# VectorE writes the attention's high part of x from the output bank, and the head's side work is spread over its steps

## The reference

```python
scores = scale * np.matmul(q, k.transpose(0, 1, 3, 2))       # 2 batches, 8 heads, 768 tokens, head size 64
keep = is_sink | in_window                                   # 4 sink tokens, window of 128
scores = np.where(keep, scores, -1000000000.0)
a = np.exp(scores - np.max(scores, axis=-1, keepdims=True))
a = a / (np.sum(a, axis=-1, keepdims=True) + 1e-09)
x = matmul(a, v), reshaped to 1536 tokens x 512
h = x @ w_in;  x = np.maximum(0.01 * h, h) @ w_out           # 512 -> 2048 -> 512
h = x @ w_in2; y = (h * (1.0 / (1.0 + np.exp(-h)))) @ w_out2
```

## Time and profile before

| what | before |
|---|---|
| median of three runs | 673.38 us (671.8 to 674.53) |
| the profiled execution's own time | 672.19 us |
| its span in the trace | 669.8 us |
| TensorE busy | 642.4 us, 96% |
| VectorE busy | 278.2 us, 42% |
| ScalarE busy | 299.9 us, 45% |
| GpSimd busy | 119.1 us, 18% |
| head, to the first hidden tile | 68.67 us |

### The profile page before, as it was taken

The page is one execution under the profiler, slowest core; times in us unless marked ns, Lnnn a source line. Parts: engine busy times, 40 slices in busy tenths (PEclk is TensorE's granted clock), DMA queues, the critical chain, the costliest instruction groups (busy, mean ns, idle before and its releaser), DMA issues.

```text
span 669.8 us, 9081 instructions
## 1 busy us (share of the span) xinstructions
PE 642.4 (96%) x3113; PEld 528.3 (79%) x3113; DVE 278.2 (42%) x646; ACT 299.9 (45%) x676; POOL 119.1 (18%) x165
## 2 busy tenths in 40 slices
PE   5989899989989999999999999999999999999997
PEld 3667688877768888887888888888888888888886
DVE  3669555555535555552222225333322222212222
ACT  3778556565536556642333335333322333223332
POOL 4767333242314233310000000000000000000000
PEclk8899999999989999999999999999999999999999
DMA  4664234334331223111011122233211111201101
GB/s 114 174 191 118 81 114 119 111 96 126 97 94 33 79 65 112 32 60 35 1 63 64 64 63 95 94 98 103 103 75 31 64 63 64 95 0 64 64 0 63
DMA packets 16940, 53.27 MB, mean 80 GB/s; under 512 B 2560, under 2 KB 2560, under 8 KB 16896
## 3 DMA queue, kind: packets, MB, share of 16 engines
q1 hardware_dynamic: 16512, 52.63, 25.9%
q10 hardware_dynamic: 384, 0.07, 0.1%
HBM read 49.55 MB, written 3.15 MB: 79 GB/s over the span
## 4 chain that ended last, share of the span: by engine, by line
PE 78%; issue 7%; DVE 5%; ACT 3%; POOL 2%; DMA 2%; POOLq 0%; SPq 0%; ACTq 0%; DVEq 0%
PE h_ps L797 36%; PE y_ps L823 33%; PE o_ps L763 3%; DMA qk_raw<-qk 2%; PE t_ps L731 2%; PE s_ps L718 1%; DVE wout L600 1%; DVE win L594 1%; ACT wout L456 1%; PE y_ps L707 1%; ACT prob L413 1%; DVE g L605 1%; DVE pT L551 1%; POOL k_hl L333 1%; PE t_ps L741 1%
## 5 line engine op out<-in xcount | busy, mean ns | idle before, releaser
L797 PE MATMUL h_ps<-x,win 128*128 128x512 f32 x1152 | 284.6, 394 | 9.1 <-DVE win L594 5.3
L797 PEld LDWEIGHTS h_ps<-x,win 128*128 128x128 f32 x1152 | 214.0, 189 | 54.2 <-DVE win L594 6.9
L463 ACT ACTIVATE g_f<-h_ps 128x512 f32<-128x512 f32 x96 | 57.4, 598 | 268.9 <-PE h_ps L797 268.7
L823 PE MATMUL y_ps<-g,wout 128*128 128x512 f32 x576 | 146.5, 395 | 1.2 <-PE o_ps L763 1.2
L823 PE MATMUL y_ps<-wout,g 128*128 128x512 f32 x576 | 138.2, 389 | 0.0
L600 DVE TENSOR_TENSOR wout<-w_raw,wout 128x512 fp32r<-128x512 f32 x64 | 47.2, 737 | 192.9 <-ACT wout L456 192.9
L823 PEld LDWEIGHTS y_ps<-wout,g 128*128 128x128 f32 x576 | 108.1, 188 | 22.4
L823 PEld LDWEIGHTS y_ps<-g,wout 128*128 128x128 f32 x576 | 103.9, 188 | 20.7 <-issue 1.9
L605 DVE TENSOR_TENSOR g<-g_f,g 128x512 fp32r<-128x512 f32 x96 | 66.0, 687 | 99.9 <-ACT g L465 99.9
L413 ACT ACTIVATE prob<-sm,neg_max 128x260 f32<-128x260 f32 (+1 forms) x96 | 47.0, 490 | 56.5 <-DVE neg_max L543 56.4
L465 ACT ACTIVATE g<-h_ps 128x512 fp32r<-128x512 f32 x96 | 56.9, 593 | 0.0
(11 more groups left out here) (76 smaller groups left out, 415.4 us busy)
## 6 DMA issues: line engine op xcount, KB each, us to landing
w_raw<-w SPq DMA_DIRECT2D x64, 512.0 KB, 3.3
qk_raw<-qk SPq DMA_DIRECT2D x48, 260.0 KB, 4.5
v_raw<-vt SPq DMA_DIRECT2D x12, 256.0 KB, 4.4
y<-qk_raw SPq DMA_DIRECT2D x12, 256.0 KB, 2.3
vs_raw<-vsink ACTq DMA_DIRECT2D x8, 8.0 KB, 4.5
```

Of the source, the lines that this page charges most:

```text
L463: nc.scalar.activation(g_f32[:, F % 2, :], h_ps[:, :], func, alpha=slope)
L797: ins = mm(h_ps[:, :], win[:, split_slot[split_of[F]], wp, c * P:(c + 1) * P], x[:, xp, c, tokens(F)], start=(c == 0 and wp == HI and xp = ...
L823: ins = mm(y_ps[d][:, :], a[:, d * P:(d + 1) * P], r, start=(first and wp == HI and gp == HI), stop=(last and wp == LO))
```

## The change

The high part of x is no longer copied from `att` by ScalarE. VectorE multiplies the output bank by `scale` twice, once into the high part of `x` (two instructions of 64 partitions that write fp32r) and once into `att`; GpSimd waits for both. In the same change:

- the four first weight loads are issued in steps 9, 11, 13 and 15 in place of 4 to 7;
- slice 0 is split in ticks -5 (win) and -3 (wout), and slice 1's win in tick -2, in place of -2, -1 and -1;
- the seven instruction groups on the sink values are set one by one into steps 3 to 9;
- filler is one matmul per step from step 8 on;
- the first half of tile 5's q and k is split in step 19 in place of 18, on ScalarE between the exponential and the first hidden tile's function.

```diff
+    first_loads = (9, 11, 13, 15)
...
-        if s < FT:
+        if s < 2:
+            at, at_out = 3 * s - 5, 3 * s - 3
+        elif s < FT:
             at, at_out = s - 2, s - 1
...
-            return 1 if T < TB else 2
+            return 1 if T < TB else 3 if T == TB else 2
...
-                if PAIRS <= a < 2 * PAIRS:
-                    load_w(a - PAIRS)
+                if a in first_loads:
+                    load_w(first_loads.index(a))
...
-                pool.wait_ge(x_high, e + 1)
+                pool.wait_ge(x_high, 2 * e + 2)
+                pool.wait_ge(att_ready, e + 1)
...
-            def high_x(e):
-                T, half = divmod(e, 2)
-                act.wait_ge(att_ready, e + 1)
-                nc.scalar.activation(x[:, 0, 2 * half:2 * half + 2, T * P:(T + 1) * P], att[:, :, :],
-                                     ACT.Copy).then_inc(x_high, 1)
...
-                if a in scaled_in:
-                    high_x(scaled_in[a])
...
                 if a == FS:
+                    high_qk(T + 1, 0)
                     take_hidden(0)
...
                 wait(dve, x_ready, e)
+                for lo in (0, D):
+                    src = o_bank(e)[lo:lo + D, :].rearrange("p (c n) -> p c n", c=2)[:, :, 2 * lo:2 * lo + P]
+                    nc.vector.tensor_tensor(x[lo:lo + D, 0, 2 * half:2 * half + 2, T * P:(T + 1) * P], src,
+                                            scale[lo:lo + D, :, :], ALU.mult).then_inc(x_high, 1)
...
-            stack_sink_values()
...
+                if 3 <= a < 3 + 5 + B:
+                    stack_sink_values(a - 3)
...
-                    fill(3)
+                    fill(3 if a < 2 * PAIRS else 1)
```

More of the change, by code:

```diff
@@ L503, in _ @@
                 if a == FS:
+                    high_qk(T + 1, 0)
                     take_hidden(0)
-                if a == FS:
                     exp(2 * a + 1)
@@ L518, in _ @@
                     evacuate(F, 0)
-                    if j == j_split(T) and T + 1 < TILES:
-                        high_qk(T + 1, 0)
+                if a > FS and j == j_split(T) and T + 1 < TILES:
+                    high_qk(T + 1, 0)
             for F in range(LAST - FS, NSTEP):
@@ L582, in scale_half @@
             def scale_half(e):
+                T, half = divmod(e, 2)
                 dve.wait_ge(o_done, e + 1)
@@ L621, in evacuate, with stack_sink_values @@
                         nc.vector.tensor_copy(out_sb[:, d, :], y_ps[d][:, :]).then_inc(out_dve, 1)
[L623 to L632, removed]
-                n = H * NS
[L634 to L637, removed]
+            def stack_sink_values(piece):
+                n = H * NS
+                if piece == 0:
+                    dve.wait_ge(vs_loaded, 16 * B * REP)
+                    nc.vector.tensor_copy(vs_hi[:, :, :], vs_raw[:, :, :]).then_inc(vs_step, 1)
+                elif piece == 1:
+                    dve.wait_ge(const_step, CONSTS)
+                    nc.vector.tensor_reduce(block_of[:, :],
+                                            ident[:, :].rearrange("p (r h s) -> p h r s", r=REP, h=H),
+                                            mybir.AxisListType.XY, ALU.add).then_inc(vs_step, 1)
+                elif piece == 2:
+                    dve.wait_ge(vs_step, 1)
+                    nc.vector.tensor_copy(vs_part[:, :, :], vs_hi[:, :, :].bitcast(F32)).then_inc(vs_step, 1)
+                elif piece < 5:
+                    dve.wait_ge(vs_step, 3)
+                    rows = slice((2 * piece - 5) * n, (2 * piece - 4) * n)
                     nc.vector.tensor_tensor(vs_part[rows, :, :], vs_raw[rows, :, :],
                                             vs_hi[rows, :, :].bitcast(F32), ALU.subtract).then_inc(vs_step, 1)
-                dve.wait_ge(vs_step, 5)
-                for b in range(B):
+                else:
+                    b = piece - 5
+                    dve.wait_ge(vs_step, 5)
                     nc.vector.tensor_tensor(vs_st[:, b, :, :],
```

## The result

The changed kernel takes 674.24 us (median of 20 runs, 671.92 to 675.87), the kernel before 672.22 us in as many runs. The ratio is 1.0025, interval 1.0015 to 1.0036: a small loss, 1.7 us by the ratio, clear of no change. The time lies inside the range of the forecast (673.0 us), but on the other side of no change: the forecast stood against 673.38 us as a slight gain. The profiled execution has a span of 672.4 us against 669.8.

What follows compares the result with a forecast made beforehand. TensorE's head was full partly by filler, the others close behind; VectorE would become the bound. Terms -0.1 (head), +0.7 (borders), +0.3 (splitting steps) made +0.9 us on 672.19: 673.1, written 673.0, range 667.5 to 678.5.

Steps and rivals of the forecast that it cites:

- VectorE becomes the bound of the head: Head, steps 9 to 18: VectorE needs about 5.9 us per two steps against 5.30 before, first hidden tile near 70.0.
- blocking: Head: eight VectorE instructions on SBUF wait for GpSimd, 0.35 each in steps 4 to 8, 0.4 after; 3.0 us in all.
- The 48 instructions on x at 0.42 us: VectorE's new instructions for the high part of x read PSUM and scale, so no blocking is added: 0.42 us each.
- The filler buys nothing: Head: with VectorE as bound, the 0.44 us of filler taken from each of eleven steps gains no time.
- The DMA stall goes, since the first weight load is issued four steps later: Head, steps 4 to 8: VectorE's 3.25 us idle piece for the late qk load disappears as loads come one by one.
- In the three steps where q and k are split on the same tick ... taken at +0.1 each: Behind the head: ScalarE up to 0.5 us earlier, GpSimd's x 0.37 later; +0.1 us each, bounds -0.5 and +0.4.
- Block borders: Two borders behind the head where TensorE waits for x: two more instructions, +0.4 us each, 0.7 together.
- I write 673.0: Whole kernel: +0.9 us on the profiled execution's 672.19 gives 673.1, written as 673.0; three runs had a median of 673.38.
- B: Faster rival: VectorE's added work goes into gaps more than allowed, without blocking; about 668 us, chance 0.25.
- C: Slower rival: eight VectorE instructions meet GpSimd's q and k often and wait the full 1.1 us; 679 us, chance 0.12.
- D: Clock rival: with less filler the granted clock falls to 1.2 GHz in the head; +14, 687 us, chance 0.03.
- E: Slower rival: behind the head 0.86 us per half delays masks and g, 16 ticks at 0.3; 678 us, chance 0.10.

Runs made afterwards that it cites:

- the third experiment: Changed kernel with ScalarE's copy of att into x for the eight halves of the head, VectorE's two instructions behind it: 670.93 us, ratio 0.9990 to the kernel before.
- that of the first: Changed kernel with ScalarE's copy of att into x again, all else of the change kept: 668.0 us, ratio 0.9943 to the kernel before.
- The fourth experiment: Changed kernel with GpSimd subtracting q and k ahead of x in the splitting ticks: 671.09 us, ratio 0.9991 to the kernel before.
- the first four experiments: Changed kernel with ScalarE's copy (668.0 us), kernel before with only x changed (678.17), changed kernel with the copy only in the head (670.93), with GpSimd's new order (671.09).

## Why the prediction was right or wrong

**VectorE becomes the bound of the head: right, and near in size.** The last scaling was to end at 69.1 us and ended at 69.07; the first hidden tile was to stand at 70.0 and stood at 70.09. Steps 4 to 8 were to take 17.3 and took 17.37, steps 9 to 18 32.9 and took 32.02. That sum is in part luck: the start gained 4.25 us at the mask of step 4, not 5.0, and blocking cost 1.4 us, not 3.0. Of the eight instructions exposed to it two were hit (0.96 for 0.29 and 1.45 for 0.68), and the three weight splits ran in 0.69 each. The two k subtractions at the start were held as I took it (1.42 and 1.52 us), and the first mask came at 10.45 for 10.8.

**The 48 instructions on x at 0.42 us: right.** Their means are 0.419 and 0.422, and none was over 0.43.

**The filler buys nothing: right,** by the runs with three filler matmuls, 1.0032 against 1.0025.

**"The DMA stall goes, since the first weight load is issued four steps later": right that it goes, not shown that the loads are the reason.** With the loads back in steps 4 to 7 the time is the same within the interval. Here the late load cost nothing once VectorE, by its added work, came later than ScalarE did behind the load.

**"In the three steps where q and k are split on the same tick ... taken at +0.1 each": the term that failed.** It was 0.3 us in the sum and measured 1.9. It was weighed as a gain of ScalarE against a delay of GpSimd of 0.37 us. Both sides were off. The delay is 0.5 us: GpSimd's x began 1.39 us after VectorE's scaling did in step 20 of the kernel before and begins 1.90 us after it now. And ScalarE's gain bought nothing in steps 24, 28 and 32: its wout stands at the same point of the tick as before, and VectorE's wout beside it waits for GpSimd's k. There k meets wout in both kernels, wout ends 0.55 us after k, and so the delay of k goes on to win and to TensorE in full: 0.47, 0.54 and 0.58 us, each over the bound of +0.4. Step 32 had no wait before, and I had left it out for that. In step 20 ScalarE's earlier wout does get VectorE past wout before k comes (0.69 in place of 1.21 us), but k then meets g (1.82 in place of 0.69), which costs 0.31. With GpSimd's order changed the term goes, which shows that the place of k is the cause.

**Block borders: right in mechanism, a little small.** 0.52 us each against 0.4; the two handovers, VectorE to GpSimd and GpSimd to TensorE, took 0.16 and 0.14 us, where I had allowed 0.2 for both.

**The sum.** +0.9 us was forecast on the profiled execution, +2.6 us came in the span: 1.6 of the 1.7 us missing are the splitting ticks, 0.3 the borders, and -0.1 the head.

**"I write 673.0": the step that turned the sign.** The sum said that the kernel gets 0.9 us longer. It was added to the 672.19 of one execution, and the result was set beside the 673.38 that three runs gave for the kernel before, so a loss by the sum was forecast as a gain of 0.4. Added to 673.38 the same sum gives 674.3. The median of 20 runs of the kernel before is 672.22, so it was the 673.38 that stood high, by 1.2 us, more than the whole effect forecast. With the splitting ticks at their measured 1.9 the sum would have been +2.5, over 673.38 from either base. By the prediction's own mark, under 0.5% is "same", the result is the outcome to which it gave 0.54.

**Rivals.** B (about 668) did not come; its time is that of the spread head without the pair on x (668.0), which is what the pair used up. C did not come: blocking was half of what was counted. D came in small: the clock fell to 0.50 for about 3 us in the profiled execution, from about 57 to 60 us, with VectorE still full. In the two microseconds from 54 to 56 TensorE had been busy 0.36 and 0.01 us. In one head with ScalarE's copy such a dip went with a first hidden tile 1.2 us later than in its twin. E, the delay behind the head, is the rival that came, in its mild form: in four ticks and two borders, not in sixteen ticks.

**Left open.** What made `pT` late in step 14 of the kernel with the sink values first. Why the change of x costs 3.4 us in the head of the kernel before and about 2.4 in the spread one: the waits and the fall of the clock are shown, but no run took them apart.

## What to carry to other kernels

Before moving work from an engine that waits to one that is busy, sum the second engine's work in the stretch: here 0.86 us per half moved the head's bound to VectorE, and with its delay in the ticks cost 5.5 us, more than the 3.8 us that the rest of the change had won. Time in which an engine stands waiting is no load that has to be moved away: with the copy left on ScalarE, and ScalarE's weight splits put ahead of its wait for `att`, the ratio was 0.9924 (0.9943 without that, with intervals that overlap, and a head 1.0 us longer in the execution without the fall of the clock). Where two engines hold each other up, follow a delay to the instruction that it meets. Here it was passed on in full where the pair met already, and changed its pair in one tick of four; an earlier instruction on a third engine did not make up for it. And when the effect is smaller than the spread of the runs, add the sum to the same number that the result will be compared with.

## What the runs showed of the hardware that was not expected

VectorE's small instructions can be held longest for their size: a subtraction on 32 partitions took 0.96 us beside GpSimd and 0.29 with nothing beside it. In steps 24, 28 and 32, before and after, VectorE's wout ended 0.54 to 0.56 us after the end of the GpSimd instruction that it met, whether wout lasted 1.05 or 1.77 us. GpSimd is held in turn, as k in step 20 shows (1.76 us, against a mean of 1.32).

TensorE's granted clock in the head, between 22 and 68 us, fell to 0.50, its low level of 1.2 GHz, in five of the eight profiled kernels that have one filler matmul per step from step 8 on: from about 57 to 60 us in the changed one, 53 to 60 in the one with ScalarE's copy, 32 to 35 with GpSimd's order changed (in part before the filler gets thinner), 59 to 62 with the sink values first and 57 to 61 with the loads early. It also fell in the kernel before with only the change of x, which has three filler matmuls in every step. In the third experiment, whose head is the same as that of the first, it did not fall, nor in the two kernels with the splits ahead of the copy. The fourth experiment's head has the changed kernel's instructions and the same hole in TensorE's work (0.06 and 0.31 us busy of the two microseconds from 54 to 56), and no fall there. So a look at one execution doesn't tell whether a kernel is free of it. The kernel before has such differences too: of its 28 executions beside the first four experiments, those with a mean granted clock of 0.994 took 670.6 to 671.9 us, those at 0.989 or less 673.5 to 675.7.
